# A gated linear recurrence with two mixture layers behind it: how the recurrence's tiles, gates and loads are laid out

## The chip, the cores and the metric

One core of a Trainium2 chip runs the whole kernel. The metric is device time in microseconds (us) from start to end of one execution. Engines are named as in the profile: PE is the matrix engine, PEld its weight loads, DVE the vector engine, ACT the scalar engine, POOL the general-purpose engine, SP the engine that only issues transfers. SPq and ACTq are the transfers that SP and ACT issue.

## The reference

For each batch b (4) and head h (8), over 768 positions t, with head size 40:

```python
m_new  = max(f[t] + m, i[t])                      # running maximum of the gate logs
f_stab = exp(f[t] + m - m_new); i_stab = exp(i[t] - m_new)
C = f_stab * C + i_stab * outer(v[t], k[t])       # state, 40 x 40
n = f_stab * n + i_stab * k[t]
y[t] = sigmoid(o[t]) * (C @ q[t]) / max(|n . q[t]|, 1)
```

Then the 3,072 rows of 320 values go through two layers. In the first, a router assigns each token to one of eight experts with room for 384 tokens each, in order of the logits; each expert is relu(x @ w1) @ w2 with hidden size 1,024. The second is one dense layer x @ w_in (hidden size 2,048), a leaky rectifier with one slope per hidden unit, and @ w_out.

## The kernel before, in words

**The recurrence** is computed by chunks of 128 positions: 6 chunks (c) times 4 batches (b) make 24 tiles, T = 4c + b, in this order. Inside a tile the recurrence becomes matrix products. For the eight heads of a tile:

- `front` (PE): the log decays (L576, called LOGD below) from the gate rows `peak3`, then the scores k.q (L583, SCORE), two heads in one product. The two heads of a pair lie on rows 0 to 39 and 64 to 103 of `k_in` and `q_wide`, so 104 rows are used; `q_wide` holds each head's q beside zeros, so that a pair shares one weight load.
- `decays` (ACT, L841) turns the log decays to weights, `make_probs` (DVE, L1016) multiplies them with the scores, and `weigh_values` (POOL, L466 to L478) weighs the values, masks the product and fades the state.
- `back` (PE): q times the carried state (L606, CARRY), the state's update (L612, UPD), the router's logits of two tiles earlier (L595), and the output (L622, YB). `turn_x` (L631) transposes the finished rows of the tile before.
- `make_x` (DVE, L1036 to L1056): adds the carried part, adds the update to the state, divides by the norm, multiplies with the output gate `sig`, and writes `x_sb`. ACT copies the transpose (L848, L849) and issues the store of x (L851, L852).

The engines run side by side and meet at semaphores. In a step for tile T, PE does front(T+1), back(T), turn_x(T-1); DVE does make_probs(T+1), make_x(T); ACT does decays(T+1), copy_xT(T-1), and in chunks 1 to 4 `high_piece`, a sixteenth of the split of the dense layer's weights into a high and a low part (L879 to L883). POOL makes the low part (`low_piece`, L486 to L494). SP issues the nine transfers of a tile (`load_tile`, L381 to L385) when the tile four before it is done with its buffers. ACT issues the raw weights of the next chunk's four pieces in one go (`load_raw`, L865 to L868).

**Ahead of the loop** DVE computes the gate logs of all 768 positions for all 32 rows (batch and head) in one go (L969 to L989), ACT exponentiates them (L825, L826), PE transposes them (L556) and spreads the per-chunk fade (L560), DVE copies the results (L996, L1000). ACT also loads the whole output gate o (six transfers) and takes its sigmoid (L821). POOL sets constants and clears the padded buffers (L418 to L456). PE waits for all of POOL's constants (`consts`, 7) before its first transpose.

**After the loop** the router's assignment is worked out, then eight experts and the dense layer run (L711 to L726 are their products). The change does not touch this part.

Of the kernel before, what the change touches and what calls it, by code (L numbers as in the profile page):

```python
# [34 lines left out]
def build_program(nc, qT, kT, k, v, o, i_gate, f_gate, w_gate, w1, w2, w_in, w_out, alpha, out):  # L35
# [13 lines left out]
    ODD = 64  # L49
    PD = ODD + D  # L50
# [18 lines left out]
    with ExitStack() as keep:  # L69
# [128 lines left out]
        q_wide = ga("q_wide", [PD, B, HP, 2, P])  # L198
        k_in = ga("k_in", [PD, B, HP, P])
        k_row = ga("k_row", [P, B, HP, PD])  # L200
        sig = ga("sig", [P, NT, DM])
# [14 lines left out]
        assert ga.at <= wi_at, (ga.at, wi_at)  # L216
# [7 lines left out]
        pre = Region(wi_at)  # L224
        gate_i = pre("gate_i", [HB, S])
        gate_f = pre("gate_f", [HB, S])
        not_first = pre("not_first", [HB, S])
        cum_f = pre("cum_f", [HB, S])
        log_in = pre("log_in", [HB, S])
        peak = pre("peak", [HB, S])  # L230
        carry = pre("carry", [HB, NCH + 1])
        g_log = pre("g_log", [HB, S])
        w_log = pre("w_log", [HB, S])
        g_row = pre("g_row", [HB, S])
        w_row = pre("w_row", [HB, S])
        neg_peak = pre("neg_peak", [HB, S])
        neg_a = pre("neg_a", [HB, S])
        neg_b = pre("neg_b", [HB, S], BF16)
        g_mid = pre("g_mid", [HB, S])
        diag = pre("diag", [HB, NCH, HB])  # L240
        ones_f = pre("ones_f", [HB, D])
# [3 lines left out]
        CARRY, UPD, YB, XTB = bank[4:8]  # L245
        ACC, UP = bank[0:3], bank[3:6]
# [12 lines left out]
        consts = sem("consts")  # L259
        pool_step = sem("pool_step")  # L260
        dve_step = sem("dve_step")
        gate_logs = sem("gate_logs")
        gate_exps = sem("gate_exps")
        peak3_ready = sem("peak3_ready")
        gates_turned = sem("gates_turned")
        gates_ready = sem("gates_ready")
        tile_in = [sem(f"tile_in{b}") for b in range(B)]
# [6 lines left out]
        o_in = [sem(f"o_in{c}") for c in range(NCH)]  # L274
        sig_ready = sem("sig_ready")
# [26 lines left out]
        raw_in = sem("raw_in")  # L302
# [52 lines left out]
        LOADS = 9 * 16  # L355

# [7 lines left out]
        def _(sp):  # L364
            sp.dma_start(gate_i[:, :], i_gate.rearrange("b h s -> (b h) s")).then_inc(gates_in, 16)
            sp.dma_start(gate_f[:, :], f_gate.rearrange("b h s -> (b h) s")).then_inc(gates_in, 16)
            sp.dma_start(wg_sb[:, 0:2, :], w_gate[0:2 * P, :].rearrange("(t p) e -> p t e", p=P),
                         allow_slow_non_contiguous=True).then_inc(consts_in, 16)
            sp.dma_start(wg_sb[0:REST, 2, :], w_gate[2 * P:DM, :]).then_inc(consts_in, 16)
            sp.dma_start(alpha_sb[:, :], alpha.rearrange("(j p) -> p j", p=P),  # L370
                         allow_slow_non_contiguous=True).then_inc(consts_in, 16)

            def load_tile(c, b):
                T = B * c + b
                if not first(T, B):

                    sp.wait_ge(y_done, T - B + 1)
                    sp.wait_ge(vw_ready, T - B + 1)
                for half, at_row in enumerate((0, ODD)):
                    rows = slice(at_row, at_row + D)  # L380
                    sp.dma_start(q_in[rows, b, :, :], qT[c, b, half]).then_inc(tile_in[b], 16)  # L381
                    sp.dma_start(q_wide[rows, b, :, half, :], qT[c, b, half]).then_inc(tile_in[b], 16)
                    sp.dma_start(k_in[rows, b, :, :], kT[c, b, half]).then_inc(tile_in[b], 16)
                    sp.dma_start(k_row[:, b, :, at_row:at_row + D], k[c, b, :, half]).then_inc(tile_in[b], 16)
                sp.dma_start(v_in[:, b, :, 0:D], v[c, b]).then_inc(tile_in[b], 16)  # L385

            sp.wait_ge(consts, 1)

            over_chunks(sp, load_tile)

# [24 lines left out]
        def _(pool):  # L416
            ch = Chain(pool, pool_step)
            pool.memset(v_in[:, :, :, D:D1], 1.0)  # L418
            pool.memset(q_in[:, :, :, :], 0.0)
            pool.memset(q_wide[:, :, :, :, :], 0.0)  # L420
            pool.memset(k_in[:, :, :, :], 0.0)
            pool.memset(k_row[:, :, :, :], 0.0)
            pool.memset(fade[:, :, :, :], 1.0)
            pool.memset(state[:, :, :, :], 0.0).then_inc(consts, 1)
            ch.mark(pool.memset(ident[:, :], 0.0))
            ch.mark(pool.memset(sel3[:, :], 0.0))
            ch.link(pool.memset(ones_bf[:, :], 1.0))
# [3 lines left out]
            for n in range(3):  # L431
                ch.link(pool.affine_select(out=sel3[:, :], in_=sel3[:, :], compare_op=ALU.not_equal, fill=1.0,
                                           base=-n * HB, pattern=[[-1, HB]], channel_multiplier=1))
            pool.memset(ones_f[:, :], 1.0).then_inc(consts, 1)

            pool.affine_select(out=upper[:, :], in_=ones_bf[:, :], compare_op=ALU.is_gt, fill=0.0, base=0,
                               pattern=[[1, P]], channel_multiplier=-1).then_inc(consts, 1)
# [8 lines left out]
                      allow_small_or_imprecise_dtypes=True).then_inc(consts, 1)  # L446

            pool.iota(route_tie[:, :, :], pattern=[[-8 * P, NCH], [-8 * S, B], [-1, E]], base=8 * 4095 + E - 1, channel_multiplier=-8,
                      allow_small_or_imprecise_dtypes=True).then_inc(consts, 1)
# [9 lines left out]
            def weigh_values(c, b):  # L459
                T = B * c + b  # L460
                n = b % 2
                pool.wait_ge(tile_in[b], LOADS * (c + 1))
# [11 lines left out]
                if final(T):  # L474
                    return
                if not first(T, 2):
                    pool.wait_ge(state_ready, T - 1)
# [22 lines left out]
            pool.wait_ge(gates_ready, 5)  # L500
# [45 lines left out]

        @block.tensor
        def _(pe):
            pe.wait_ge(consts, 7)

            pe.wait_ge(gate_logs, 1)
            for n, row in enumerate((log_in, g_row, w_row)):
# [802 lines left out]
```

## Time and profile before

| | |
|---|---|
| median of 3 runs | 937.66 us (932.39 to 949.05) |
| profiled execution: its time / its span | 934.4 us / 932.4 us |
| mean granted PE clock | 0.926 of full speed |
| busy: PE, PEld, DVE, ACT, POOL | 89%, 84%, 62%, 34%, 17% |
| packets moved | 102,514, of them 67,984 under 512 B |

The span is the time from the first to the last instruction of the profiled execution. The clock is a share of 2.4 GHz: 1.00 is 2.4 GHz and 0.50 is 1.2 GHz; a value between is a stretch that holds both. Busy shares are means over parts of the kernel with quite different limits. The parts are: the set-up up to 21.7 us, the recurrence up to 218 us, the assignment up to about 260 us, and the two layers from there to the end.

### The profile page before, as it was taken

How to read it: one execution, taken by the hardware profiler on the slowest of the kernel's cores; microseconds unless marked ns; L12 is line 12 of the kernel's file. 1: busy time of each engine (PE TensorE's matmuls, PEld its weight loads, DVE VectorE, ACT ScalarE, POOL GpSimd, SP SyncE). 2: the span in 40 equal slices, each digit the busy share in tenths (PEclk: the TensorE clock that was granted, in tenths of full speed). 3: DMA queues.
4: the chain of work that ended last, by engine and by line, in shares of the span. 5: the costliest groups of instructions: out<-in, count | busy, mean ns of one | idle time of the engine just before them, and what ended most of it. 6: DMA issues, size and time to landing. Idle time of an engine off the chain costs nothing.

```text
span 932.4 us, 19545 instructions
## 1 busy us (share of the span) xinstructions
PE 834.0 (89%) x6878; PEld 785.1 (84%) x6878; DVE 580.3 (62%) x1405; ACT 319.8 (34%) x732; POOL 163.0 (17%) x233
## 2 busy tenths in 40 slices
PE   1979999995379989998999999899989989998995
PEld 1879899994269979998998899799989979998995
DVE  7648546765765775677567657756765775676342
ACT  5435435540032351343135123413432351343231
POOL 6427545720000011011001100110110011011001
PEclk9989668985579999998999899999999999999999
DMA  9687755620320410050023004000500310050000
GB/s 249 159 205 187 172 126 145 150 69 18 95 67 2 130 33 23 1 156 26 0 63 98 21 0 135 25 21 0 160 21 0 116 45 21 0 152 30 1 1 21
DMA packets 102514, 68.58 MB, mean 74 GB/s; under 512 B 67984, under 2 KB 92048, under 8 KB 102480
## 3 DMA queue, kind: packets, MB, share of 16 engines
q1 hardware_dynamic: 85872, 45.05, 19.0%
q10 hardware_dynamic: 13920, 14.42, 5.2%
q0 software_dynamic: 2688, 8.65, 2.9%
q8 instruction: 21, 0.34, 0.2%
q14 instruction: 13, 0.11, 0.0%
HBM read 59.46 MB, written 8.65 MB: 73 GB/s over the span
## 4 chain that ended last, share of the span: by engine, by line
PE 52%; DVE 19%; issue 11%; ACT 8%; SPq 4%; DMA 2%; POOL 1%; ACTq 1%; DVEq 0%; POOLq 0%
PE bank L711 10%; PE bank L712 8%; PE bank L713 8%; DVE g_act L1242 7%; ACT h_hi L932 5%; PE bank L658 5%; PE bank L583 4%; PE bank L622 4%; PE bank L725 2%; PE bank L606 2%; DVE w_lo L1225 2%; PE bank L726 2%; PE bank L595 2%; PE bank L612 1%; DMA s<-w 1%
## 5 line engine op out<-in xcount | busy, mean ns | idle before, releaser
L711 PE MATMUL bank<-wo_hi,h_hi 128*128 128x320 f32 x384 | 122.8, 320 | 0.6 <-DVE h_lo L1245 0.6
L932 ACT CAST h_hi<-g_act 128x384 fp32r<-128x384 f32 x128 | 65.6, 513 | 167.2 <-DVE g_act L1242 167.2
L713 PE MATMUL bank<-wo_hi,h_lo 128*128 128x320 f32 x384 | 120.4, 314 | 0.0
L712 PE MATMUL bank<-wo_lo,h_hi 128*128 128x320 f32 x384 | 119.9, 312 | 0.0
L1245 DVE TENSOR_TENSOR h_lo<-g_act,h_hi 128x384 fp32r<-128x384 f32 x128 | 71.5, 559 | 74.1 <-ACT h_hi L932 74.1
L520 POOL DMA_INDIRECT xe<-x_rows,idx_in x24 | 28.7, 1196 | 473.9 <-DVE idx_in L1188 418.7
L928 ACT ACTIVATE h_hi<-bank 128x384 fp32r<-128x384 f32 x64 | 31.5, 492 | 186.1 <-PE bank L726 186.1
L1242 DVE SCALAR_TENSOR_TENSOR g_act<-g_neg,rest_alpha,bank 128x384 f32<-128x384 f32 x128 | 78.2, 611 | 26.8 <-ACT g_neg L930 24.8
L711 PE MATMUL bank<-yT_hi,wi_hi 128*128 128x384 f32 x256 | 90.6, 354 | 0.1
L712 PE MATMUL bank<-yT_lo,wi_hi 128*128 128x384 f32 x256 | 86.8, 339 | 0.0
L713 PE MATMUL bank<-yT_hi,wi_lo 128*128 128x384 f32 x256 | 86.6, 338 | 0.0
L930 ACT ACTIVATE g_neg<-bank 128x384 f32<-128x384 f32 x128 | 62.6, 489 | 56.9 <-PE bank L726 55.8
L711 PEld LDWEIGHTS bank<-wo_hi,h_hi 128*128 128x128 f32 x384 | 73.7, 192 | 0.9 <-DVE h_lo L1245 0.9
L713 PEld LDWEIGHTS bank<-wo_hi,h_lo 128*128 128x128 f32 x384 | 73.7, 192 | 0.0
L712 PEld LDWEIGHTS bank<-wo_lo,h_hi 128*128 128x128 f32 x384 | 73.7, 192 | 0.0
L658 PEld LDWEIGHTS bank<-choice,by_row 128*128 128x128 bf16 x1920 | 54.3, 98 | 22.7 <-issue 7.7
L658 PE MATMUL bank<-choice,by_row 128*128 128x8 bf16 x1920 | 61.7, 167 | 11.2 <-DVE by_row L1114 6.7
L711 PE MATMUL bank<-h_hi,w_hi 128*128 128x384 f32 x192 | 69.8, 363 | 0.0
L712 PE MATMUL bank<-h_lo,w_hi 128*128 128x384 f32 x192 | 64.9, 338 | 0.0
L713 PE MATMUL bank<-h_hi,w_lo 128*128 128x384 f32 x192 | 64.7, 337 | 0.0
L583 PE MATMUL bank<-q_wide,k_in 104*128 104x256 f32 x192 | 59.5, 464 | 1.3 <-DVE probs L1016 1.3
L531 POOL DMA_INDIRECT out<-out_sb,idx_out x24 | 24.5, 1020 | 191.9 <-DVE out_sb L1305 187.0
(198 smaller groups left out, 1831.2 us busy)
## 6 DMA issues: line engine op xcount, KB each, us to landing
s<-w SPq DMA_DIRECT2D x8, 1280.0 KB, 9.2
s<-w SPq DMA_DIRECT2D x8, 1024.0 KB, 5.2
s<-w SPq DMA_DIRECT2D x24, 256.0 KB, 6.4
sig<-o ACTq DMA_DIRECT2D x6, 640.0 KB, 8.3
q_in<-qT SPq DMA_DIRECT2D x48, 80.0 KB
q_wide<-qT SPq DMA_DIRECT2D x48, 80.0 KB
k_in<-kT SPq DMA_DIRECT2D x48, 80.0 KB
k_row<-k SPq DMA_DIRECT2D x48, 80.0 KB
```

What stands on the lines that cost most here:

```text
L520: pool.indirect_dma_start(xe[:, t, :], None, x_rows[:, :], bass.IndirectOffsetOnAxis(ap=idx_in[:, t:t + 1], axis=0)).then_inc(rows_in, 16)
L583: ins = pe.matmul(SCORE[y // 2][:, 2 * P * (y % 2):2 * P * (y % 2) + 2 * P], k_in[:, b, y, :], q_wide[:, b, y, :, :].rearrange("p u t -> p ...
L622: ins = pe.matmul(YB[:, D1 * h:D1 * h + D1], probs[:, n, half, y, :], v_in[:, b, h, :], start=True, stop=True)
L658: ins = pe.matmul(CNT[n], above_full(c), choice[:, c, :], start=(n == 0 and c == 0), stop=(c == NT - 1), skip_group_check=True)
L711: pe.matmul(acc, ah, bh, start=start, stop=False, skip_group_check=True)
L712: pe.matmul(acc, ah, bl, start=False, stop=False, skip_group_check=True)
L713: return pe.matmul(acc, al, bh, start=False, stop=stop, skip_group_check=True)
L928: act.activation(h_hi[:, k % 3, :], acc, ACT.Relu).then_inc(act_ready, 1)
L930: act.activation(g_neg[:, k % 3, :], acc, ACT.Relu, scale=-1.0).then_inc(act_ready, 1)
L932: act.copy(h_hi[:, k % 3, :], g_act[:, k % 3, :]).then_inc(g_hi, 1)
L1242: dve.scalar_tensor_tensor(out=g_act[:, n, :], in0=g_neg[:, n, :], scalar=rest_alpha[:, j:j + 1], in1=acc, op0=ALU.mult, op1=ALU.add).then ...
L1245: dve.tensor_tensor(h_lo[:, n, :], g_act[:, n, :], h_hi[:, n, :].bitcast(F32), ALU.subtract).then_inc(h_ready, 1)
```

## The change

Everything happens in the part up to 218 us and in what feeds it.

- **Rows.** The head pair lies on 80 adjacent rows (`PD = 2 * D`) instead of 104. `k_row` becomes the plain rows of k (320 wide), pairs are heads n and n+2 of a group of four, and the state's update multiplies with `own_half`, a 0/1 column for each half, over all 80 rows, instead of adding on 40 rows twice. `q_in` is filled by two transfers in the new pair order, `k_in` by one instead of two, `k_row` by one instead of two.
- **Gates chunk by chunk.** Ahead of the loop only chunk 0's gates are made. The gates of chunk c+1 are made beside chunk c: DVE `gate_sums` after make_x of b = 0, `split_peak` and `fade_weights` after b = 1, `copy_gates` in make_x of b = 2; ACT `gate_weights` at b = 1; PE `turn_gates` in back of b = 2, ahead of YB. In the first chunk nothing is faded, and the state is written without an old one.
- **Output gate.** o is loaded per tile into `gate_o`; ACT takes tanh(o/2) in place per tile, and DVE computes (1 + tanh) times the scaled row, with the norm doubled.
- **Raw weights.** SP issues them, two transfers per step (each for two of the four pieces of a chunk), behind the tile's own loads, instead of ACT once per chunk.
- **Set-up.** POOL's order is new: only what the first tile needs comes first, buffers `k_in`, `q_in`, `k_row`, `state`, `fade` are no longer cleared, DVE clears `q_wide` of batch 0. The router weights are loaded after tile 1. The eleven small DVE operations that prepare constants of the assignment (`setup`) move to the step of tile 20.

```diff
+            def gate_sums(c):
...
+                gc.link(dve.tensor_tensor_scan(cum_f[:, :], ones_row[:, :], gate_f[:, cs], 0.0, ALU.mult, ALU.add))
+                gc.link(dve.tensor_tensor(log_in[:, :], gate_i[:, cs], cum_f[:, :], ALU.subtract))
+                gc.link(dve.tensor_tensor_scan(peak[:, :], log_in[:, :], log_in[:, :], carry[:, 0:1], ALU.max, ALU.max))
+                gc.link(dve.tensor_tensor(g_log[:, :], carry[:, 0:1].to_broadcast([HB, P]), peak[:, :], ALU.subtract))
+                dve.tensor_tensor(w_log[:, :], log_in[:, :], peak[:, P - 1:P].to_broadcast([HB, P]), ALU.subtract).then_inc(gate_logs, 1)
+                gc.link(dve.tensor_tensor(carry[:, :], cum_f[:, P - 1:P], peak[:, P - 1:P], ALU.add))
...
+            def split_peak(c):
...
+                gc.link(dve.tensor_scalar(neg_peak[:, :], peak[:, :], -1.0, None, ALU.mult))
+                gc.link(dve.tensor_copy(peak3[0:HB, cs], neg_peak[:, :]))
+                gc.link(dve.tensor_tensor(neg_a[:, :], neg_peak[:, :], peak3[0:HB, cs], ALU.subtract))
+                gc.mark(dve.tensor_copy(peak3[HB:2 * HB, cs], neg_a[:, :]))
+                gc.link(dve.tensor_copy(neg_b[:, :], neg_a[:, :]))
+                gc.link(dve.tensor_tensor(g_mid[:, :], neg_a[:, :], neg_b[:, :], ALU.subtract))
+                dve.tensor_copy(peak3[2 * HB:3 * HB, cs], g_mid[:, :]).then_inc(peak3_ready, 1)
...
+            def fade_weights(c):
+                dve.wait_ge(gate_exps, c + 1)
+                dve.tensor_scalar(fade_diag[:, :], ident[0:HB, 0:HB], g_row[:, P - 1:P], None, ALU.mult).then_inc(diag_ready, 1)
...
+            def turn_gates(c):
...
+                pe.wait_ge(gate_exps, c + 1)
+                if not first(c, 1):
+                    pe.wait_ge(diag_ready, c)
+                    pe.transpose(GATES[1], g_row[:, :], ident[0:HB, 0:HB])
+                    for half in range(2):
+                        pe.matmul(FADE, half_ones[:, half, :], fade_diag[:, :].rearrange("p (g n u) -> p n g u", n=2, u=2)[:, half, :, :],
+                                  start=(half == 0), stop=(half == 1), skip_group_check=True)
+                pe.transpose(GATES[0], log_in[:, :], ident[0:HB, 0:HB])
+                pe.transpose(GATES[2], w_row[:, :], ident[0:HB, 0:HB]).then_inc(gates_turned, 1)
...
                     router(*prev(c, b, 2))
+                if b == 2 and not final(T):
+                    turn_gates(c + 1)
...
+            def gate(c, b):
+                T = B * c + b
+                act.wait_ge(o_in[b], 16 * (c + 1))
+                act.activation(gate_o[:, b, :], gate_o[:, b, :], ACT.Tanh, scale=0.5).then_inc(tanh_ready, 1)
...
             def load_tile(c, b):
...
+                sp.dma_start(k_in[:, b, :, :], kT[c, b].rearrange("u d y s -> (u d) y s")).then_inc(qk_in[b], 16)
+                if first(T, B):
+                    sp.wait_ge(*((wide_zero, b) if b else (wide_zero0, 1)))
+                for half in range(2):
+                    sp.dma_start(q_wide[D * half:D * half + D, b, half, :, :], qT[c, b, half]).then_inc(qk_in[b], 16)
+                sp.dma_start(k_row[:, b, :], k[c, b].rearrange("p u y d -> p (u y d)")).then_inc(kv_in[b], 16)
+                sp.dma_start(v_in[:, b, :, 0:D], v[c, b]).then_inc(kv_in[b], 16)
+                if not first(T, B):
+                    for half in range(2):
+                        sp.dma_start(q_in[D * half:D * half + D, b, :, :].rearrange("d (a u) s -> d a u s", u=2),
+                                     qT[c, b].rearrange("u d (a n) s -> n d a u s", n=2)[half]).then_inc(q_rows_in[b], 16)
+                    sp.wait_ge(x_ready, T - B + 1)
+                sp.dma_start(gate_o[:, b, :], o[T]).then_inc(o_in[b], 16)
...
+            def load_raw(c, b):
...
+                if b % 2 == 0:
+                    sp.dma_start(wi_raw[:, :, fs], w_in[0:2 * P, fs].rearrange("(t p) f -> p t f", p=P)).then_inc(raw_in[b], 16)
...
+                else:
+                    sp.dma_start(rest_raw[0:REST, fs], w_in[2 * P:DM, fs]).then_inc(raw_in[b], 16)
+                    sp.dma_start(rest_raw[REST:P, fs], w_in[2 * P:DM, fs]).then_inc(raw_in[b], 16)
...
             def step(c, b):
...
+                if b == 0 and not final(T):
+                    gate_sums(c + 1)
+                if b == 1 and not final(T):
+                    split_peak(c + 1)
+                    fade_weights(c + 1)
+                if isinstance(T, int) and T == NT - B:
+                    setup()
```

## Rows read from the trace of the kernel before

**Rows 1.** Busy time by stretch: stretch, length, busy of each engine (instructions), clock, DMA

```profile
0.00:21.70 21.70, 2.88 (x22) 2.28 (x22) 15.44 (x33) 12.71 (x11) 14.07 (x39) 1.00 0.92 256
21.70:218.00 196.30, 187.57 (x1304) 174.77 (x1304) 116.71 (x287) 85.48 (x305) 94.24 (x138) 0.84 0.61 147
...
98.70:146.30 47.60, 47.57 (x233) 43.77 (x234) 22.72 (x58) 16.79 (x60) 22.26 (x33) 0.57 0.60 141
```

**Rows 2.** Order of time in the set-up: start us, length us, what [idle before, releaser]

```profile
6.29 1.75 DVE L969 TENSOR_TENSOR_SCAN cum_f<-not_first,gate_f 32x768 f32<-32x768 f32 x1 [4.34 <-DMA gate_f<-f_gate]
...
15.35 0.85 PE L556 MATMUL bank<-ident,log_in 32*128 32x32 f32 x6 [15.35 <-POOL steps L456]
...
21.73 1.01 PE L576 MATMUL bank<-peak,sel 96*128 96x128 bf16 x8 [0.75 <-issue]
```

**Rows 3.** Transfers: what, queue, count, KB each, us from issue to landing

```profile
gate_i<-i_gate SPq DMA_DIRECT2D x1, 96.0 KB, 3.0
```

**Rows 4.** Set-up by line: operation, count, busy us, mean ns, idle before

```profile
L821 ACT ACTIVATE sig<-sig 128x1280 f32<-128x1280 f32 x6 | 7.3, 1261 | 0.2 <-DMA sig<-o 0.2
L975 DVE TENSOR_TENSOR_SCAN peak<-log_in,carry 32x128 f32<-32x128 f32 x6 | 2.9, 491 | 0.2
L821 ACT ACT_TABLE_LOAD x2 | 2.6, 1283 | 6.3 <-issue 6.3
...
L985 DVE TENSOR_TENSOR neg_a<-neg_peak,peak 32x768 f32<-32x768 f32 x1 | 0.9, 946 | 0.0
...
L976 DVE TENSOR_TENSOR carry<-cum_f,peak 32x1 f32<-32x1 f32 x6 | 0.9, 147 | 0.2
```

**Rows 5.** Order of time, PE's first products of tile 5

```profile
53.37 1.03 PE L576 MATMUL bank<-peak,sel 96*128 x8 [4.30 <-DMA v_in<-v]
...
54.20 3.63 PE L583 MATMUL bank<-q_wide,k_in 104*128 104x256 f32 x8
```

**Rows 6.** Order of time in one step at full clock, PE alone

```profile
179.31 1.95 PE L583 MATMUL bank<-q_wide,k_in 104*128 104x256 f32 x8
...
181.94 0.90 PE L612 MATMUL bank<-vw,k_row 128*104 128x82 f32 x8
...
183.47 1.98 PE L622 MATMUL bank<-v_in,probs 128*128 128x41 f32 x16
...
186.08 1.95 PE L583 MATMUL bank<-q_wide,k_in 104*128 104x256 f32 x8
```

**Rows 7.** The same step on DVE, POOL, ACT and SP's queue

```profile
178.81 0.50 DVE L1036 TENSOR_TENSOR carried<-bank,gT 128x328 f32<-128x328 f32 x1 [0.85 <-PE bank L622]
...
180.73 0.84 DVE L1051 TENSOR_SCALAR norm<-nq 128x8 f32<-128x8 f32 x1
...
182.91 0.50 DVE L1056 TENSOR_TENSOR x_sb<-scaled,sig 128x320 f32<-128x320 f32 x1 [0.25 <-DVE scaled L1053]
183.45 1.28 DVE L1016 TENSOR_TENSOR probs<-decay,bank 128x512 f32<-128x512 f32 x2
...
180.67 0.87 POOL L486 TENSOR_TENSOR wo_lo<-wo_raw,wo_hi  x1 [1.22 <-ACT wo_hi L879]
...
181.22 2.13 ACT L841 ACTIVATE decay<-bank,aT 128x128 f32<-128x128 f32 x8
...
179.06 0.79 SPq L382 DMA_DIRECT2D q_wide<-qT  x1
...
183.18 0.60 SPq L385 DMA_DIRECT2D v_in<-v  x1
```

**Rows 8.** Order of time behind the raw weights' issues of a chunk

```profile
66.28 0.46 ACT L879 CAST wo_hi<-wo_raw  x1 [3.34 <-issue]
...
69.75 0.40 PE L576 MATMUL bank<-peak,sel 96*128 x4 [0.38 <-ACT decay L841]
```

**Rows 9.** Order of time, LOGD of two steps in the low-clock stretch

```profile
110.82 1.06 PE L576 MATMUL bank<-peak,sel 96*128 x8
...
120.77 1.06 PE L576 MATMUL bank<-peak,sel 96*128 x8
```

More of the change, by code:

```diff
@@ L301, in build_program @@
         stage2_in = sem("stage2_in")
-        raw_in = sem("raw_in")
+        raw_in = [sem(f"raw_in{b}") for b in range(B)]
         prep_hi = sem("prep_hi")
@@ L392, in _ @@
+            with sp.Fori(1, NCH - 1) as c:
+                for b in range(B):
+                    load_tile(c, b)
+                    load_raw(c, b)
+            for b in range(B):
+                load_tile(NCH - 1, b)
             sp.wait_ge(y_done, NT)
@@ L417, in _ @@
             ch = Chain(pool, pool_step)
[L418 to L426, printed above, removed]
@@ new lines, in _ @@
+            for b in range(2, B):
+                pool.memset(q_wide[:, b, :, :, :], 0.0).then_inc(wide_zero, 1)
+            ch.mark(pool.memset(half_ones[:, :, :], 0.0))
+            ch.link(pool.memset(own_half[:, :], 1.0))
+            for half in range(2):
+                pool.memset(half_ones[:, half, D * half:D * half + D], 1.0)
+            ch.mark(pool.affine_select(out=own_half[:, 0:1], in_=own_half[:, 0:1], compare_op=ALU.is_gt, fill=0.0,
+                                       base=D, pattern=[[0, 1]], channel_multiplier=-1))
@@ L894, in _ @@
                     high_piece(c, b)
-            for b in range(B):
-                step(NCH - 2, b)
-                high_piece(NCH - 2, b)
             for b in range(B):
@@ new lines, in _, with setup @@
+            gate_sums(0)
+            split_peak(0)
+            dve.wait_ge(gates_turned, 1)
+            gc = gate_chain(0, LOG_LINKS + PEAK_LINKS)
+            gc.mark(dve.tensor_copy(aT[:, 0, :], GATES[0]))
+            gc.mark(dve.tensor_copy(wT[:, 0, :], GATES[2]))
+            gc.link(dve.tensor_copy(gT[:, 0, :], GATES[0]))
+            dve.sem_inc(gates_ready, 1)
+            def setup():
+                ch = Chain(dve, setup_step)
+                dve.wait_ge(consts, 5)
+                dve.wait_ge(consts_in, 48)
+                ch.mark(dve.tensor_scalar(rest_alpha[:, :], alpha_sb[:, :], -1.0, 1.0, ALU.mult, ALU.add))
+                for n in range(NS - 1, -1, -1):
+                    ch.link(dve.tensor_scalar(steps[:, n, :], steps[:, 0, :], float(2 ** STEPS[n][1]), None, ALU.mult))
@@ L1032, in make_x @@
                 dve.wait_ge(y_done, T + 1)
+                if b == 2 and not final(T):
+                    copy_gates(c + 1)
+                if b == 0 and not first(T, 1):
+                    dve.wait_ge(gates_ready, c + 1)
                 if first(T, B):
```

298 lines of the change are left out of this document (142 added, 156 removed).

## The prediction

> **What bounds the kernel now.** I read the busy time by stretch first, then the order of time in each, then the lines for prices. Three stretches matter here. Up to 21.7 us PE is busy for 2.88 us and the transfer engines for 0.92 of the time: DVE, ACT and POOL prepare, PE waits. From 21.7 to 218 us, the recurrence, PE is busy for 187.57 of 196.3 us. Within it, from 98.7 to 146.3 us, the clock is 0.57 [rows 1]. Behind 218 us nothing is changed, and I carry those 714 us over.
>
> One step at full clock shows what sets its pace: SCORE starts at 179.31 and the next tile's at 186.08, so 6.77 us, and PE is busy throughout [rows 6]. DVE is a close second. It starts on the tile's output at 178.81, writes x at 182.91 to 183.41, then makes the next weights until 184.73. That is 5.92 of 6.77 us [rows 7]. SCORE at 186.08 needs these weights, so they come 1.35 us early. That slack is the number on which most of this rests.
>
> **The set-up.** PE's first transpose waits for POOL until 15.35, and LOGD starts at 21.73. DVE's chain can't start before 6.29, because it waits 4.34 us for gate_f [rows 2]. gate_i, one issue ahead of it, landed after 3.0 us [rows 3]. After the change ACT no longer moves the whole of o at that time. I take 3.0 us also for gate_f, issued at about 1.3: landing at 4.3. The other end is 6.3, as now. Then DVE does chunk 0 alone. A scan of 128 columns is 0.49. An operation of 768 columns is 0.95 and one of a single column 0.15, so one of 128 columns is about 0.28 [rows 4]. gate_sums is two scans, three such operations, the carry and 0.2 of gaps: 0.98 + 0.84 + 0.15 + 0.2 = 2.2 us. split_peak is seven at 0.28 at most, with gaps 2.2 us. LOGD then starts at 4.3 + 4.4 = 8.7 instead of 21.7: **13.0 us less** (11 to 14). POOL has less to clear and PE needs only two of its constants, so POOL drops out of the chain. The ACT table and the weights' exponential run beside split_peak.
>
> **The wait for tile 5's loads** goes. PE waits 4.30 us for v_in at 53.37 and then does SCORE in 3.63 instead of 1.95, at the low clock [rows 5, 6]. Before it, the transfer engines had carried o, nine transfers per tile and a whole chunk of raw weights at once. After it, o comes by tile, k as rows of 1,280 bytes instead of 160, and raw weights in halves. That is 4.3 + 1.7, **6.0 us less** (0 to 6.5; nothing if another transfer is late there).
>
> **Raw weights off ACT.** In the step where ACT issues four transfers its next work starts 3.34 us late, the decays follow, and PE waits 0.38 in LOGD and a little more ahead of SCORE [rows 8]. I take 0.7 for each of the two issues at full clock: **1.4 us less** (0 to 3). What would be late next is SP. A step has four transfers with the cut of q_wide (0.79 each) and up to six like v_in (0.60) [rows 7]: 6.8 us of issuing at the very most, with the short ones nearer 0.4 some 6 us. It fits the step only just. x_ready, for which SP now waits ahead of gate_o with the raw loads queued behind it, comes 4.6 us into the step, when SP has got there anyway. A tile's loads have some two steps to land, so a small overrun is covered; if that cover is gone, each step costs what SP is over.
>
> **The state's update** loads 80 columns of weights instead of 104. PE spends 0.90 us on it, its end overlapping the next [rows 6]. Were it all weight loading, 24/104 of it, 0.2 us, would go; were it the 82 moving columns, nothing. I take 0.07 per step and 20 steps: **1.5 us less** (0 to 4). SCORE, CARRY and YB have the columns they had, so fewer rows give nothing. DVE's two state operations cover 80 rows instead of 40 with 164 columns as before: nothing.
>
> **tanh per tile.** 1,280 columns took 1.26 us [rows 4]; 320 take about 0.45. ACT's decays end at 183.35, next to x at 183.41 [rows 7], so with tanh they become the later of the two by 0.4, out of 1.35 of slack: no cost in a plain step.
>
> **setup** moves eleven operations of 0.15 to 0.28 into the step of tile 20. DVE has 0.85 us idle there, and 0.65 more since no state is written: **1.5 us more** (0 to 3).
>
> **The gates beside the loop** are the large term. Let YB of tile 4c end at 0, which is 178.67 in the step shown. DVE writes x at 4.74, now does gate_sums until 6.9, and makes the next weights until 8.2. SCORE of tile 4c+3 was due at 7.4: PE waits 0.8. make_x of the next tile starts at 8.2 and takes 4.6, then split_peak and fade_weights take 2.5: 15.3. PE does SCORE from 8.2 and would start YB 4.16 later (183.47 less 179.31), at 12.3. There turn_gates stands in front of it and waits for fade_weights: 3.0 us, with YB queued behind. Its own three transposes at 0.14 (six take 0.85 [rows 2]) and two small products make 0.7. In sum **4.5 us per chunk** at full clock. copy_gates puts 0.7 us ahead of the carried part, whose reader on PE has 1.2 us: nothing. At the low clock a step takes 9.95 us (110.82 to 120.77 [rows 9]) and hides all but the 0.7 and a little, say 1.5. With three of five chunks at full clock, as now, it is 3 x 4.5 + 2 x 1.5 = 16.5, and as the small operations are priced at their upper end I take **16 us more** (3.5, PE's own work alone, to 22.5).
>
> POOL can make this worse. The norm, an operation on 8 columns, takes 0.84 us at 180.73 and ends just as POOL's 0.87 us subtraction does [rows 7], where a small operation takes 0.15 [rows 4]: DVE is held while POOL reads. Caught once in each of two bursts, in three chunks at full clock, that is 6 x 0.7 = 4 us. The Trainium skill, SBUF — State Buffer (section "SBUF: two separate sides"), has the rule: DVE and GpSimd share a pair of ports by an exclusive lock that is held for a whole instruction. By that rule the sum would be 4 us higher than by free ports.
>
> **Sum.** The profiled execution took 934.4 us. 934.4 - 13.0 - 6.0 - 1.4 - 1.5 + 1.5 + 16 = **930 us**. It lies 3.3 under the median of the three runs, less than the clock's own swing below, so I leave it there. Under 2% is about what a measurement of this kernel can't tell from no change: 918.9 to 956.4 counts as the same.
>
> **The rivals.**
>
> 1. *The low clock doesn't come back.* In the stretch at 0.57 five steps cost up to 3.2 us each more than at full clock, with waits about 20 us. It began in a step behind ACT's issues, at 98.7, and these go. Against: turn_gates makes PE wait each chunk, and the clock also fell where PE waited for v_in [rows 5]. Then 930 - 20, and + 6 for the gate work fully paid in five chunks: 916 (903 to 922).
> 2. *DVE takes in the gates.* If the bursts meet gaps, only PE's 0.7 per chunk stays: 930 - 12.5 = 918. For it: 116.71 us busy in 196.3 [rows 1]. Against: the gaps are those of the low clock; at full clock 0.85 us per step are left for 7.5 us per chunk of four.
> 3. *The clock falls at every gate wait* (slower). Place: turn_gates at b = 2. Price: 3.2 us per step until the clock is back. With three low steps in each of five chunks it is 15 x 3.2 = 48 us, where 20 are counted already, and the gate waits are hidden (-12.5): 930 + 15 = 945 (940 to 961). It decides for slower than before from about twelve low steps on. For it: SCORE ran at the low clock behind PE's wait of 4.30 [rows 5]. Against: after the wait of 0.38 at 69.75 LOGD still took 0.40 for four products, half of 1.06 for eight at the low clock being 0.53 [rows 8, 9].
> 4. *DVE is held by POOL* in the bursts, as worked out: 934.
>
> **Chances.** Forecast 0.40 (922 to 940), rival 1 0.24, rival 2 0.10, rival 3 0.15, rival 4 0.05, rival 5 0.06. The range is 908 to 950: out of it are about a quarter of rival 1, half of rival 3's upper part and most of rival 5, some 0.18. Faster by over 2%: most of rivals 1 and 2 and a trace of the forecast, 0.29. Slower by over 2%: a quarter of rival 3 and half of rival 5 and what I don't see, 0.09. The same: 0.62. The forecast's own range is 922 to 940.
>
> **What would show it.** LOGD's first row near 8.7 us. No row of PE with a wait for a transfer behind 20 us, and no idle "issue" ahead of L879's copy. In chunks 0 to 4, PE's transposes of turn_gates with some 3 us idle before them, released by DVE's fade row, and SCORE of b = 3 with 0.8 released by the probs row. A plain step of 6.7 us. One ACT_TABLE_LOAD for the recurrence. It is wrong if DVE's step with gate_sums is not over 6.8 us, if SP's queue has no idle time, or if the granted clock over the recurrence lies far from 0.84.

## The result and the profile after

The changed kernel takes 1024.19 us (median of 4 runs, 1022.45 to 1026.62), the kernel before 942.96 us in the same session. The ratio is 1.0955, 95% interval 1.0888 to 1.1023. I forecast 930 us, 908 to 950: wrong in sign and far outside the range. Ratios, here and below, are made from the faster runs of each kernel alone, and the kernel before itself ranges from 918 to 964 us over the sessions, so a ratio can differ by about a per cent from that of the medians beside it.

The set-up went as forecast. In order of time (start us, length us, what, idle before and releaser), the rows that answer to [rows 2]:

```profile
3.57 0.41 DVE L1013 TENSOR_TENSOR_SCAN cum_f<-ones_row,gate_f 32x128 f32<-32x128 f32 x1 [1.44 <-DMA gate_f<-f_gate]
...
7.79 1.03 PE L617 MATMUL bank<-peak,sel 96*128 96x128 bf16 x8 [1.49 <-DVE peak L1031]
```

LOGD starts at 7.79 instead of 21.73 us. Busy time by stretch (as [rows 1]) shows where more than that is lost:

```profile
0.00:7.80 7.80, 0.40 (x3) 0.29 (x3) 4.87 (x17) 1.59 (x2) 6.41 (x29) 1.00 0.63 167
7.80:306.00 298.20, 295.81 (x1333) 272.96 (x1333) 138.69 (x379) 95.58 (x338) 93.73 (x147) 1.00 0.40 108
306.00:350.00 44.00, 13.63 (x283) 11.10 (x283) 30.66 (x97) 3.20 (x4) 3.59 (x3) 1.00 0.28 85
350.00:1023.30 673.30, 634.45 (x5275) 601.69 (x5275) 417.23 (x990) 218.23 (x413) 51.09 (x53) 0.98 0.15 45
```

The recurrence lasts 298.2 us instead of 196.3, and PE has only 2.4 us of idle time in it. The assignment lasts 44.0 us for 42.0, and the two layers 673.3 us where the same stretch of before, from 260.0 us on, has 672.4. PE is busy for 295.81 us with 1,333 products where it was for 187.57 with 1,304 [rows 1]. One plain step on PE, to hold against [rows 6] and [rows 9]:

```profile
209.16 3.73 PE L625 MATMUL bank<-q_wide,k_in 80*128 80x256 f32 x8
212.68 1.84 PE L652 MATMUL bank<-state,q_in 80*128 80x82 f32 x8
214.31 1.30 PE L659 MATMUL bank<-vw,k_row 128*80 128x82 f32 x8
215.40 1.46 PE L637 MATMUL bank<-wg_sb,xT_sb 128*128 128x8 f32 x6
216.79 3.63 PE L670 MATMUL bank<-v_in,probs 128*128 128x41 f32 x16
220.22 0.88 PE L679 MATMUL bank<-ident,x_sb 128*128 128x128 f32 x3
220.90 1.06 PE L617 MATMUL bank<-peak,sel 96*128 x8
221.75 1.59 PE L625 MATMUL bank<-q_wide,k_in 80*128 80x256 f32 x3
```

A step takes 12.59 us where [rows 6] had 6.77. Every product is slow, also one whose shape the change leaves alone: the output's (L670) takes 3.63 against 1.98, much as the score's takes 3.73 against 1.95. That is a halved clock, not a slower SCORE. It holds through all 24 tiles. One line of source, all its products (durations in ns: least, median, most; first and last start in us), after and then before:

```profile
L625 PE MATMUL bank<-q_wide,k_in x192: 634/634/793, 8.6 to 286.6; 80*128 80x256 f32 x192
```

```profile
L583 PE MATMUL bank<-q_wide,k_in x192: 379/379/797, 22.5 to 201.4; 104*128 104x256 f32 x192
```

Before, the shortest product took 379 ns and so did the median one. After, not one of 192 is under 634.

The record of the granted clock says 1.00 for 7.8 to 306 us in the rows above, and 0.984 for the whole run. The durations contradict it. In the kernel before, the same length stands beside a record of 0.50, in the stretch 131.6 to 143.6 us (SCORE in order of time, then the busy time of the stretch); the step that fills it takes 12.9 us, LOGD starting at 130.74 and the next at 143.63:

```profile
121.63 3.73 PE L583 MATMUL bank<-q_wide,k_in 104*128 104x256 f32 x8
...
131.59 3.73 PE L583 MATMUL bank<-q_wide,k_in 104*128 104x256 f32 x8
```

```profile
131.60:143.60 12.00, 12.00 (x51) 11.16 (x50) 3.68 (x10) 3.39 (x12) 4.65 (x7) 0.50 0.91 203
```

In this stretch the clock had been high and fallen again. Ahead of its first rise in the loop the record reads 1.00 in the kernel before too: so it does from 20 to 30 us, where the first SCORE, at 22.54, takes 3.73. So from here on I read the clock from SCORE: eight products in 1.95 us are 2.4 GHz, in 3.73 us 1.2 GHz. By that reading the whole recurrence after runs at 1.2 GHz. The Trainium skill, TensorE: Matmul & The Clock Gate (Part 1), warns that the recorded clock events have been seen to be unreliable; this trace agrees.

PE's waits within the recurrence are all of this (what it waited for, us in total, times, longest):

```profile
PE bank L617 <- DVE peak L1031: 1.5, 1, 1.5
PE bank L637 <- ACT xT_sb L897: 0.7, 1, 0.7
PE bank L625 <- DVE probs L1073: 0.6, 1, 0.6
PE bank L652 <- DVE hsum L1098: 0.4, 1, 0.4
```

The first is the end of the set-up, where PE waits for chunk 0's gates. Inside the loop none is a wait for gates or for a transfer. Nothing stops PE, and yet it never reaches the clock that it had before.

### The profile page after: what moved, and what is told of

Same layout as the page of the kernel before. It is cut to its first block, busy times and chain, and to the rows that moved or that the text cites. A ratio compares the mean times of both kernels' runs of the same rounds, so it can differ in the third digit from the quotient of the medians.

```text
span 1023.3 us, 19916 instructions
## 1 busy us (share of the span) xinstructions
PE 944.3 (92%) x6893; PEld 886.0 (87%) x6893; DVE 591.5 (58%) x1482; ACT 318.6 (31%) x756; POOL 154.8 (15%) x231
## 4 chain that ended last, share of the span: by engine, by line
PE 62%; DVE 18%; issue 10%; ACT 7%; DMA 1%; DVEq 0%; SPq 0%; POOL 0%; ACTq 0%; POOLq 0%
PE bank L759 9%; PE bank L670 8%; PE bank L625 8%; PE bank L760 8%; PE bank L761 8%; DVE g_act L1319 6%; ACT h_hi L968 5%; PE bank L706 5%; PE bank L652 3%; PE bank L637 3%; PE bank L659 2%; PE bank L617 2%; PE bank L773 2%; PE bank L774 2%; DVE w_lo L1302 2%
## 5 line engine op out<-in xcount | busy, mean ns | idle before, releaser
L625 PE MATMUL bank<-q_wide,k_in 80*128 80x256 f32 x192 | 89.5, 648 | 0.6 <-DVE probs L1073 0.6
L670 PE MATMUL bank<-v_in,probs 128*128 128x41 f32 x384 | 87.1, 416 | 0.0
L670 PEld LDWEIGHTS bank<-v_in,probs 128*128 128x128 f32 x384 | 83.8, 330 | 0.7
L625 PEld LDWEIGHTS bank<-q_wide,k_in 80*128 80x128 f32 x192 | 61.7, 336 | 13.8 <-DVE probs L1073 0.9
```

The source lines that it names most:

```text
L625: ins = pe.matmul(SCORE[y // 2][:, 2 * P * (y % 2):2 * P * (y % 2) + 2 * P], k_in[:, b, y, :], q_wide[:, b, :, y, :], start=True, stop=True)
L670: ins = pe.matmul(YB[:, D1 * h:D1 * h + D1], probs[:, n, half, y, :], v_in[:, b, h, :], start=True, stop=True)
```

## The experiments

**Theory 1:** SCORE now reads 80 rows instead of 104, and how many rows it reads decides whether the clock rises. **Rivals:** the gates' stops bring it down (rival 3 of the prediction); or another part of the change, such as CARRY's 80 rows or the order of the loads.

Ratios below are to the kernel before in the same session, with their 95% interval. A kernel with no ratio beside its time was run once.

### The rows given back: 128 rows

```diff
-        q_wide = ga("q_wide", [PD, B, 2, HP, P])
-        k_in = ga("k_in", [PD, B, HP, P])
+        q_wide = ga("q_wide", [P, B, 2, HP, P])
+        k_in = ga("k_in", [P, B, HP, P])
...
+                pool.memset(k_in[:, b, :, :], 0.0)
...
-... k_in[:, b, y, :], q_wide[:, b, :, y, :] ...
+... k_in[0:P, b, y, :], q_wide[0:P, b, :, y, :] ...
```

> The changed kernel, but k_in and q_wide have 128 rows, rows 80 to 127 cleared ahead of the first load, and SCORE runs over 128 rows instead of 80 (the same columns, the same result). Theory 1 (the clock of the recurrence hangs on how many rows of PE the SCORE products use): SCORE comes back to 1.95 us in most tiles, a step to 6.7 to 7.5 us, and the time to 915 to 940. Theory 2 (the clock stays low because the chunk-wise gates make PE wait and the early start has other timing): SCORE stays at 3.73, time 1022 to 1028. Theory 3 (it is the order in which q_wide is read, two stretches instead of one): as theory 2, 1022 to 1028.

Measured: 941.38 us (936.39 to 950.51), before 943.51; ratio 1.0002 [0.9954, 1.005]. All 83 us are back, though rows 80 to 127 hold zeros, so that no product gets another value. Clearing them costs 0.9 us of set-up (the first SCORE starts at 9.54 for 8.62). This kernel is no faster than the kernel before, but that one has 104 rows; the two are set side by side at equal rows behind the last experiment.

```profile
L627 PE MATMUL bank<-q_wide,k_in x192: 379/478/794, 9.5 to 210.2; 128*128 128x256 f32 x192
```

### The rows alone, in the kernel before

```diff
-... k_in[:, b, y, :], q_wide[:, b, y, :, :] ...
+... k_in[0:80, b, y, :], q_wide[0:80, b, y, :, :] ...
```

> The kernel before, with SCORE over rows 0 to 79 of its 104 (leaves 24 rows out of the scores, so the result is not the reference's). All else, gates up front, loads, waits, is the kernel before. Theory 1: the clock never rises in the recurrence, all 24 SCORE groups near 3.73 us, a step near 12.7 us, the recurrence some 300 us long instead of 196, time 1030 to 1045. Theories 2 and 3: no change, 930 to 950.

Measured: 1045.12 us. The kernel leaves rows 80 to 103 out of the scores, so its result is not the reference's; its instructions are otherwise the same. With nothing else of the change, SCORE over 80 rows costs the kernel before some 100 us:

```profile
L583 PE MATMUL bank<-q_wide,k_in x192: 634/634/792, 22.5 to 301.3; 80*128 80x256 f32 x192
```

This and the kernel above are the two halves of the proof: the rows without the rest give the loss, the rest without the rows gives none. The order in which `q_wide` is stored, which the change alters too, is the old one here, so it is not the cause either.

### How many rows it takes

The kernel with 128 rows, with SCORE reading 0 to 103 or 0 to 95 of them:

```diff
-... k_in[0:P, b, y, :], q_wide[0:P, b, :, y, :] ...
+... k_in[0:104, b, y, :], q_wide[0:104, b, :, y, :] ...      (0:96 in the other)
```

> As the kernel with SCORE over 128 rows, but SCORE reads rows 0 to 103 of the padded buffers, the number of rows that the kernel before had. Theory 1: the clock comes and goes as in the kernel before, so 920 to 960, with some SCORE groups at 3.73 and some at 1.95. Theories 2 and 3: 1022 to 1028.

> As the kernel with SCORE over 128 rows, but SCORE reads rows 0 to 95. Theory 1a (the number of rows decides, smoothly): between 80 and 104 rows, some tiles high and most low, 960 to 1000. Theory 1b (it needs more than three quarters of the array's rows, so 96 is as 80): all 24 tiles low, 1020 to 1030. Theory 1c (anything over 80 is enough): 940 to 955.

| rows that SCORE reads | time, us | SCORE: least/median ns | last SCORE starts |
|---|---|---|---|
| 80 (the change) | 1024.19 | 634/634 | 286.6 |
| 96 | 984.25 | 379/634 | 251.4 |
| 104 | 954.72 | 379/634 | 221.7 |
| 128 | 941.38 | 379/478 | 210.2 |

The loss is graded; the kernels with 96 and 104 rows were run once each. With 96 and 104 rows the clock rises in part of the tiles, with 80 in none.

### CARRY's rows

```diff
-        state = ga("state", [PD, B, HP, 2 * D1])
-        q_in = ga("q_in", [PD, B, HP, P])
+        state = ga("state", [P, B, HP, 2 * D1])
+        q_in = ga("q_in", [P, B, HP, P])
```

> The kernel with SCORE over 128 rows, and CARRY over 128 rows too: state and q_in have 128 rows, cleared once by POOL in the set-up (3 us more there). Theory 1, if all products count and not SCORE alone: fewer low groups than with SCORE alone, time 0 to 15 us under it. If SCORE alone decides: the same time as it, within 3 us. Theories 2 and 3: 1022 to 1030.

Measured: 942.74 us, ratio 1.0006 [0.9965, 1.0048]. CARRY's rows, given back on top of SCORE's, bring nothing that can be measured; an effect of under some 4 us would not show in this interval.

### Are the gates' stops needed for the loss?

The gates of chunks 1 to 5 are made in one batch beside tiles 0 to 2, with nothing left out, once with SCORE's 80 rows and once with 128:

```diff
+            def rest_sums():
...
+                rc.link(dve.tensor_tensor_scan(r_cum[:, :], not_first[:, :], gate_f[:, rs], 0.0, ALU.mult, ALU.add))
...
-                if b == 0 and not final(T):
-                    gate_sums(c + 1)
-                if b == 1 and not final(T):
-                    split_peak(c + 1)
-                    fade_weights(c + 1)
-                if b == 2 and not final(T):
-                    turn_gates(c + 1)
+                if isinstance(T, int) and T == 2:
+                    (15 transposes and the fade products of all five chunks)
```

> The changed kernel with its 80 rows in SCORE, and the gates of chunks 1 to 5 in one batch beside tiles 0 to 2: no stop of a later chunk for gates is left. Theory 1 (the rows that SCORE reads decide the clock by themselves): every group of eight SCORE products still takes 3.7 us, and only the stops go (about 1.0 for turn_gates and 1 to 3 of waits in each of five chunks): 1010, 1000 to 1020. Rival (the 80 rows only make the clock fall because the gates stop the products chunk by chunk; my prediction's third rival): with the stops gone the clock stays high from about tile 4 on and the time is 910 to 935.

Measured with 80 rows: 1024.53 us. No gate stop is left after tile 2, and the clock is as low as ever, which refutes rival 3 as the cause of the loss. The kernel before with 80 rows says the same, since all its gates are made ahead of the loop.

```profile
L651 PE MATMUL bank<-q_wide,k_in x192: 634/634/795, 8.3 to 284.9; 80*128 80x256 f32 x192
```

My 1010 was a miss all the same. I had counted on stops that the changed kernel, at the low clock, does not have (see its waits above). The transposes and fade products of the five chunks take 2.6 us in one place (the step at 32.77 us lasts 13.53 where one without them lasts 10.97) instead of 1.0 in each of five, but SCORE of tile 1 now waits 1.5 us instead of 0.6. The last SCORE starts 1.7 us sooner, and that is all.

> The changed kernel with SCORE over 128 rows (k_in and q_wide padded with zeros), but the gates of chunks 1 to 5 are made in one batch beside tiles 0 to 2 (long rows of 640 columns, one scan for the forget sums, five for the peaks) instead of chunk by chunk; nothing is left out. Theory 1 (what the gates beside the loop cost is the stop ahead of the tiles behind b=3, and the low products that follow it): with the stops gone the later tiles run as in the kernel without gates, whose median was 907; the batch keeps the first three or four tiles low and stops them once, 3 to 10 us. 912, 900 to 922. Rival (it is the gates' work itself, on VectorE and ScalarE beside the products, wherever it stands): no faster than the kernel with gates moved inside the chunk, 932 to 941.

Measured with 128 rows: 911.75 us (907.62 to 918.25, 6 runs), before 933.78; ratio 0.9862 [0.979, 0.9934]. It computes all that the change computes and is some 110 us faster than the changed kernel. Against the kernel before it gains 1.4%, with an interval clear of 1. In order of time, SCORE's groups:

```profile
28.20 1.95 PE L653 MATMUL bank<-q_wide,k_in 128*128 128x256 f32 x8
...
98.83 3.73 PE L653 MATMUL bank<-q_wide,k_in 128*128 128x256 f32 x8
108.49 2.74 PE L653 MATMUL bank<-q_wide,k_in 128*128 128x256 f32 x8
115.91 1.95 PE L653 MATMUL bank<-q_wide,k_in 128*128 128x256 f32 x8
...
173.76 3.73 PE L653 MATMUL bank<-q_wide,k_in 128*128 128x256 f32 x8
```

Nine of 24 groups take over 2 us, four of them 3.7; in the kernel with the gates chunk by chunk it is 14. The last SCORE starts at 176.9 us instead of 210.2. The low group at 98.83 has no stop ahead of it, as the stretch up to it shows:

```profile
50.00:100.00 50.00, 50.00 (x410) 47.73 (x409) 36.30 (x92) 31.13 (x109) 35.10 (x49) 0.94 0.81 222
```

What makes the clock fall there is open.

### What the gates beside the loop cost once the clock can rise

The kernel with 128 rows, without the gates of chunks 1 to 5; cleared tiles stand in for them, so its result is not the reference's:

```diff
-                if b == 2 and not final(T):
-                    turn_gates(c + 1)
...
-                if b == 0 and not final(T):
-                    gate_sums(c + 1)
-                if b == 1 and not final(T):
-                    split_peak(c + 1)
-                    fade_weights(c + 1)
...
+            dve.memset(peak3[:, P:S], 0.0)
+            for t in (aT, gT, wT):
+                dve.memset(t[:, 1:NCH, :], 0.0)
```

> The kernel with SCORE over 128 rows, without the gates of chunks 1 to 5: gate_sums, split_peak, fade_weights, gate_weights, turn_gates and copy_gates are left out for them, and cleared tiles stand in for their gates (so the result is not the reference's). In the kernel with SCORE over 128 rows PE waits 10.3 us ahead of turn_gates in five places and 4.1 us for the late weights in four, and turn_gates takes some 0.7 us each: 18 us in all. Theory 1 (these stops also lower the clock, since the SCORE behind them is at 3.7 us each time): 18 us and 15 to 35 us of clock less, 890 to 910, SCORE at 1.95 in 20 or more tiles. Theory 2 (the stops cost what they show, the clock comes and goes by itself): 941 less 18, 918 to 928.

Measured: 906.57 us (897.27 to 909.31), ratio 0.9655 [0.9589, 0.9722], so the gates of five chunks cost 33 us by the ratios and 35 by the medians. The batch above, whose last SCORE starts at 176.9 us against 166.5 without gates and 210.2 with them in each chunk, gives most of it back with nothing left out (911.75 us). Part of the cost are stops. PE's waits in the kernel with gates and 128 rows:

```profile
PE bank L599 <- issue: 10.3, 5, 2.9
...
PE bank L627 <- DVE probs L1076: 4.1, 4, 1.2
```

L599 is turn_gates' first transpose, five times, at most 2.9 us; L627 is SCORE behind gate_sums, and 1.0 of its 4.1 us is there without the gates as well. turn_gates' own work is 0.96 us in the rows below (138.90 to 139.86), 4.8 in five chunks. In sum 10.3 + 3.1 + 4.8 = 18 us, which leaves 15 to 17. These lie in the clock. In order of time, one chunk:

```profile
131.72 3.59 PE L627 MATMUL bank<-q_wide,k_in 128*128 128x256 f32 x8 [1.25 <-DVE probs L1076]
...
138.90 0.28 PE L599 MATMUL bank<-ident,g_row 32*128 32x32 f32 x1 [1.46 <-issue]
...
139.86 3.64 PE L672 MATMUL bank<-v_in,probs 128*128 128x41 f32 x16
...
144.82 3.73 PE L627 MATMUL bank<-q_wide,k_in 128*128 128x256 f32 x8
148.34 1.17 PE L654 MATMUL bank<-state,q_in 80*128 80x82 f32 x8
...
150.72 2.44 PE L672 MATMUL bank<-v_in,probs 128*128 128x41 f32 x16
...
154.47 3.73 PE L627 MATMUL bank<-q_wide,k_in 128*128 128x256 f32 x8
```

Behind each of turn_gates' five stops, of 1.4 to 2.9 us, the output and the next SCORE run low: from the start of the one to the product behind the other PE needs 7.7 to 8.5 us (here 139.86 to 148.34), against 4.4 at 2.4 GHz, so 3.3 to 4.1 us more each time and 19 in all. That is more than the 15 to 17 left over, because the kernel without gates has falls of its own: 6 of its 24 groups take over 2 us, for 14 with the gates. Then the clock rises again: CARRY at 148.34 takes 1.17 us, where it takes 1.02 at 2.4 GHz and 1.84 at 1.2. The low group at 154.47 is a new fall inside the output at 150.72, with no stop ahead of it, so not every low group belongs to a stop. Of the four waits ahead of SCORE the two of 1.2 us were followed by a low group, those of 1.0 and 0.6 were not; and in the batch kernel SCORE at 15.62 took 1.99 us right behind a wait of 1.50. A stop makes a fall likely, not certain. In the kernel without these gates, the plain step at 2.4 GHz is 6.62 us, and whole groups are low only twice (at 82.92 and 140.79):

```profile
48.59 1.95 PE L627 MATMUL bank<-q_wide,k_in 128*128 128x256 f32 x8
55.21 1.95 PE L627 MATMUL bank<-q_wide,k_in 128*128 128x256 f32 x8
```

### The stops made smaller inside the loop

First gate_sums two chunks ahead and the peak's split in two parts, then also the fade's row one step earlier:

```diff
+            split_rest(0)
...
+            gate_sums(1)
...
-                    gate_sums(c + 1)
...
+                    split_rest(c + 1)
+                if b == B - 1 and not final(T):
+                    gate_sums(c + 2)
...
+                    fade_weights(c + 1)        (behind b = 0; only in the second kernel)
```

> The kernel with SCORE over 128 rows, the gates of the next chunk made earlier and in smaller pieces: gate_sums(c+2) after b = 3 (chunk 1's in the set-up), the first three operations of split_peak after b = 0, the other four and fade_weights after b = 1, gate_weights on ACT at b = 0; turn_gates and copy_gates where they were. Same result. The wait ahead of turn_gates should go from 2.1 us to under 0.3 per chunk, and that of SCORE stay under 1. If the stops lower the clock: 10 us and 5 to 20 of clock less, 910 to 930. If not: 930 to 935.

> The kernel with the gates early, with fade_weights moved from behind b = 1 to behind b = 0, since its row ended just as PE's first gate transpose began (63.49 and 63.59). Theory 1 (PE waits for fade_weights, DVE being late after make_x): the wait ahead of turn_gates goes from 9.1 us in five places to under 1, PE is not stopped there, and with the clock higher behind it the time goes from 937 to 910 to 925. Theory 2 (the wait belongs to turn_gates itself, PE having to stand still for it): the waits stay at 1.8 each, 930 to 940.

Measured: 936.81 us, ratio 0.9959 [0.9917, 1.0001], and 931.72 us, ratio 1.0002 [0.996, 1.0044] (the kernel before has 934.63 in the second's session). Neither gains what was expected. The first keeps 9.1 of the 10.3 us of waits at turn_gates. The second has none left there, so it was the fade's row that PE waited for, but its scores wait instead:

```profile
PE bank L627 <- DVE probs L1085: 6.7, 5, 1.9
```

DVE, POOL and SCORE, in order of time, in one burst of gate_sums:

```profile
70.63 0.86 POOL L525 TENSOR_TENSOR wo_lo<-wo_raw,wo_hi  x1 [1.37 <-ACT wo_hi L922]
70.73 1.11 DVE L1137 SCALAR_TENSOR_TENSOR x_sb<-gate_o,scaled 128x320 f32<-128x320 f32 x1
71.55 0.87 POOL L529 TENSOR_TENSOR wi_lo<-wi_raw,wi_hi  x1
71.76 0.93 DVE L1018 TENSOR_TENSOR_SCAN cum_f<-ones_row,gate_f 32x128 f32<-32x128 f32 x1
...
73.35 0.47 DVE L1020 TENSOR_TENSOR_SCAN peak<-log_in,carry 32x128 f32<-32x128 f32 x1
73.85 0.74 POOL L506 TENSOR_TENSOR vw<-v_in,wT 128x328 f32<-128x328 f32 x1 [0.68 <-POOL wi_hi L533]
73.86 0.87 DVE L1021 TENSOR_TENSOR g_log<-carry,peak 32x128 f32<-32x128 f32 x1
74.76 0.28 DVE L1022 TENSOR_TENSOR w_log<-log_in,peak 32x128 f32<-32x128 f32 x1
...
77.11 3.78 PE L627 MATMUL bank<-q_wide,k_in 128*128 128x256 f32 x8 [1.87 <-DVE probs L1085]
```

A scan took 0.93 us beside POOL's subtraction and the next one 0.47 without, a small subtraction 0.87 and 0.28; the last operation of make_x, just ahead of the burst, took 1.11 beside POOL where it takes 0.49 at 81.06. This is rival 4: these three are held for about 0.5 to 0.6 us each, 1.7 of the 1.87 by which SCORE is late, and SCORE then runs at 1.2 GHz. The Trainium skill, SBUF — State Buffer ("SBUF: two separate sides"), has the lock behind it, held by one of the two for a whole instruction, and these rows agree.

### SCORE in two halves

Half of SCORE moves between the router's products and YB, in the kernel above, in the changed kernel with 80 rows, and in the kernel before with 128:

```diff
+                score(c, b, 0)
...
+                if not isinstance(T, int) or T + 1 < NT:
+                    score(*nxt(c, b), 1)
```

> The kernel with fade_weights early, with SCORE cut in two: the products of the first four heads where they were, those of the other four between the router's products and YB of the same step. Theory 1 (the clock falls where PE does nothing with many columns for a long stretch, as YB, the transposes and LOGD are): the clock stays high nearly throughout, 22 or more tiles with SCORE at half of 1.95 per half, 895 to 910. Theory 2 (what counts is PE standing still, not what it does): the same as the kernel it starts from, within 5 us, or up to 10 more where DVE now waits for the later half.

> The changed kernel as it is, 80 rows, with SCORE cut in two in the same way. Theory 1 (80 rows are too few for the clock to rise however they are placed): all low, 1015 to 1030. Theory 2 (it is the placing of the work): some tiles high, 940 to 1000.

> The kernel before with SCORE over 128 rows, and SCORE cut in two in the same way; gates up front, raw weights on ACT as in the kernel before. Theory 1 (placing of the work keeps the clock high): no low stretch but behind the wait for the loads of tile 5, 905 to 918. Theory 2: 925 to 932.

Measured: 930.96 us, ratio 1.0072 [1.003, 1.0113]; 1023.85 us, all products low; 918.68 us, ratio 0.9875 [0.9772, 0.9979]. With 80 rows the order does not matter. For the last, the kernel before with SCORE over 128 rows and no split is the control:

> The kernel before, with q_wide and k_in on 128 rows instead of 104 and SCORE over all 128 (rows 104 to 127 cleared with the others, same result). Theory 1 (the more rows SCORE uses, the more of the time the clock is high): fewer groups at 3.7 us than in the kernel before, 910 to 930, ratio 0.97 to 0.99. Theory 2 (104 rows are enough, and the low stretches have to do with where PE waits): 935 to 948, ratio 0.995 to 1.005.

Measured: 928.37 us (922.25 to 931.72), ratio 0.9861 [0.9801, 0.9922]. Two buffers declared with 128 rows for 104 make the kernel before 1.4% faster.

```diff
-        q_wide = ga("q_wide", [PD, B, HP, 2, P])
-        k_in = ga("k_in", [PD, B, HP, P])
+        q_wide = ga("q_wide", [P, B, HP, 2, P])
+        k_in = ga("k_in", [P, B, HP, P])
```

The split adds nothing to that ratio. Its median is 10 us lower, but so is that of the kernel before in its session (934.63 for 944.20). So the split is shown to help nowhere.

With this control the rest of the change can be read at equal rows. At 128 rows it makes the kernel 1.4% slower, some 13 us (1.0002 against 0.9861, two intervals that don't meet). At 104 rows it is 954.72 us, one run, against 943.51, which points the same way but lies within the range of the kernel before. At 80 rows it is 1024.19 us against 1045.12, so 21 us faster: with the clock low throughout, the gates make PE wait for nothing, and the set-up's 14 us are most of the gain.

## Why the prediction was wrong

**The step that failed** is the sentence "SCORE, CARRY and YB have the columns they had, so fewer rows give nothing". At a given clock it holds: eight products take 3.73 us with 80 rows, with 104 and with 128 alike. But the clock is not given. With 80 rows it does not rise in any tile, which costs 83 us here (1024.19 against 941.38) and 100 alone in the kernel before (1045.12). I weighed the clock only by waits, in rivals 1 and 3, and no case had it stay low with PE busy. The prediction said that it would be wrong if the granted clock lay far from 0.84; it does, and the record hides it. The Trainium skill, TensorE: Matmul & The Clock Gate ("Why this matters for your kernels"), says that a single product over 32 rows takes as long as one over 128. The rows agree for one product at one clock, and the time of the kernel shows that more hangs on it.

**The set-up**: forecast 13.0 us less, measured 13.9 (7.79 for 21.73). Right, by the forecast's own steps: gate_f took 2.2 us to land for 3.0, and DVE 4.2 from there for 4.4.

**Tile 5's loads**: the wait of 4.3 us is gone in every variant of the changed kernel; no wait of PE in the loop is for a transfer. What that saves through the clock can't be separated.

**Raw weights, SP's queue**: in the changed kernel SP waited 119.0 us for PE ahead of `k_in`'s loads, in 20 places, but that is at steps of 12.6 us. In the kernel with 128 rows and no gates in the loop, where most steps take 6.62, it waited 8.6 us in three places and hardly had time to spare; still no wait of PE was for a transfer. So the issues fit the step only just, as forecast. The 1.4 us themselves were not isolated.

**The state's update**: 0.74 us for 0.90, and its follower starts 0.58 later instead of 0.73, so 0.15 per step and 3 us in twenty; I had 1.5. The plain step is 6.62 us for 6.77.

**tanh**: 24 operations of 473 ns, forecast 0.45, and one table load, in the set-up, for the whole recurrence. Rival 5 is refuted.

**setup**: forecast 1.5 us more. With 128 rows SCORE's last wait for DVE is at 131.72 us, so these operations, beside tile 20, made no SCORE late.

**The gates beside the loop**: forecast 16 us, with waits at turn_gates of 3.0 and at SCORE of 0.8. At the high clock the waits were at most 2.9 and 1.2, and waits and own work came to 18 us: that arithmetic was about right. At the low clock of the changed kernel they cost PE about 1.0 per chunk (a step of 13.6 for 12.6) and no wait, as forecast for low steps and as rival 2 had it. But the stops cost as much again in clock, 33 to 35 us in all. That is rival 3's mechanism. It is real, and the sum had 16 us where it measured some 34: a second mis-sized term, which eats the gain. With 128 rows, -13.9, -3 and +34 are measured, -6 and -1.4 are still the forecast's, and 24 rows more than before are worth some -13 (0.9861). That adds up to -3, and the kernel is indeed about where it was, at 1.0002.

**The low step** was priced wrongly too. The 9.95 us of [rows 9] are of a step that ran partly at 2.4 GHz, as its output would have told, with 2.52 us where 3.63 is low throughout:

```profile
117.78 2.52 PE L622 MATMUL bank<-v_in,probs 128*128 128x41 f32 x16
```

A step wholly at 1.2 GHz takes 12.6 to 12.9, so 6 us more than a high one, not 3.2. Even a rival with all 24 steps low would have come out too short by these prices: 930 - 20 - 12.5 + 24 x 3.2 = 974.

## What to carry to other kernels

Before you narrow a product that fills much of PE's time, ask what it does to the clock, and compare the same product's shortest and median time before and after. Here rows of zeros, which cost 0.9 us, bought 83. When a PE-bound kernel gets slower with PE still busy and no new wait, look at an unchanged product first: if it too takes twice as long, no dependence is to blame. And put small work that stops PE in one place rather than in every chunk: stops of 1.4 to 2.9 us cost 3.3 to 4.1 us more at half clock behind each. Last, compare two kernels at an equal number of rows before you say what the rest of a change is worth.

## What the runs showed of the hardware that was not expected

- The number of rows that one product reads changes how long PE runs at 2.4 GHz: 1024 us at 80, 984 at 96, 955 at 104, 941 at 128. Rows of zeros count. CARRY's rows, in a product half as long, did not measurably count (1.0006). Why rows count is open.
- The record of the granted clock read 1.00 through 298 us in which every product had its 1.2 GHz length, as it does ahead of the loop's first rise in the kernel before. So the mean clock in the profile of the changed kernel, 0.984, is higher than the 0.926 of the kernel before, which takes 8% less time.
- The clock also falls with PE never idle (ahead of the groups at 98.83 us in the batch kernel and at 82.92 us in the one without gates). No run here shows why.
